# Row factors turned in 32x32 blocks, low parts stacked in the last key block, score tiles halved across two banks

## What is computed

```python
scores = scale * np.matmul(q, k.transpose(0, 1, 3, 2))      # 4 batches x 8 heads, 576 x 576, D = 64
a = np.exp(causal(scores) - rowmax); a /= a.sum(-1) + 1e-09
local = np.matmul(a, v)
mem_ret  = np.einsum('bhsd,bhde->bhse', phi(q), M_prev)      # phi(x) = where(x > 0, x, exp(x) - 1) + 1
mem_norm = np.einsum('bhsd,bhd->bhs', phi(q), z_prev) + 1e-6
x = g * mem_ret / mem_norm + (1 - g) * local                # g = sigmoid(beta), one number per head
x = act1(x @ w_in1) @ w_out1                                # 2304 tokens, 512 -> 2048 -> 512
x = act2(x @ w_in2) @ w_out2                                # the same shape again
```

## Time and profile before

| | us |
|---|---|
| runs | 1031.84, 1031.50, 1033.06 |
| median | 1031.84 |
| profiled execution | 1034.39 |
| its span | 1032.6 |
| slots 0 to 5 (no dense layer) | 0 to 53.7 |
| slots 6 to 32, attention and first layer | 53.7 to about 528 |
| dense layers alone | about 528 to the end |
| granted TensorE clock, mean | 0.996 |

### The profile page before, as it was taken

How to read it: one execution, slowest core, us unless ns; L and a number is a source line. 1 busy time by engine, 2 the same in 40 slices (tenths; PEclk the granted TensorE clock), 3 DMA queues, 4 the chain that set the end, 5 groups by cost and what they waited for, 6 DMA issues and landing times.

```text
span 1032.6 us, 16556 instructions
## 1 busy us (share of the span) xinstructions
PE 1011.8 (98%) x6158; PEld 873.2 (85%) x6158; DVE 432.8 (42%) x1091; ACT 526.6 (51%) x1144; POOL 425.4 (41%) x380
## 2 busy tenths in 40 slices
PE   7889999999999999999999999999999999999997
PEld 4668888989898898988999998888888888888896
DVE  6677756656555655556531337212121211211111
ACT  6668777777676766767643456222222222322221
POOL 3367746455546455464532258322222222222211
PEclk9999999999999999999999999999999999999999
DMA  5655333323322322322201066000200200100010
GB/s 142 166 167 175 56 85 63 79 63 71 87 58 61 85 69 67 78 61 74 62 15 42 22 220 188 1 21 1 62 21 0 62 21 1 37 25 1 1 41 21
DMA packets 96272, 66.34 MB, mean 64 GB/s; under 512 B 72064, under 2 KB 85824, under 8 KB 96192
## 3 DMA queue, kind: packets, MB, share of 16 engines
q1 hardware_dynamic: 95328, 62.14, 23.4%
q10 hardware_dynamic: 864, 3.15, 1.0%
HBM read 54.53 MB, written 10.66 MB: 63 GB/s over the span
## 4 chain that ended last, share of the span: by engine, by line
PE 87%; POOL 1%; issue 0%; DVE 0%; POOLq 0%; ACT 0%
PE Hp L630 13%; PE Hp L631 12%; PE Hp L632 12%; PE Yp L653 7%; PE Yp L655 6%; PE Yp L654 6%; PE At L654 6%; PE At L655 6%; PE At L653 6%; PE At L570 5%; PE At L545 4%; PE At L494 4%; PE At L530 1%; PE At L582 0%; POOL WAl L1219 0%
## 5 line engine op out<-in xcount | busy, mean ns | idle before, releaser
L1224 POOL TENSOR_TENSOR Gl<-Gl_raw,Gh 128x512 fp32r<-128x512 f32 x144 | 191.7, 1331 | 425.7 <-ACT Gh L869 425.7
L630 PE MATMUL Hp<-Xh,WAh 128*128 128x256 f32 (+1 forms) x704 | 217.5, 309 | 1.3 <-POOL WAl L1219 1.3
L631 PE MATMUL Hp<-Xl,WAh 128*128 128x256 f32 (+1 forms) x704 | 212.5, 302 | 0.0
L632 PE MATMUL Hp<-Xh,WAl 128*128 128x256 f32 (+1 forms) x704 | 212.5, 302 | 0.0
L1085 DVE TENSOR_TENSOR Gl_raw<-Hp,Gl_raw 128x512 f32<-128x512 f32 x72 | 49.8, 692 | 296.4 <-ACT Gl_raw L861 296.3
L861 ACT ACTIVATE Gl_raw<-Hp 128x512 f32<-128x512 f32 x72 | 43.1, 598 | 230.5 <-PE Hp L632 230.5
L630 PEld LDWEIGHTS Hp<-Xh,WAh 128*128 128x128 f32 x704 | 133.2, 189 | 12.8 <-issue 2.0
L869 ACT ACTIVATE Gh<-Gl_raw 128x512 fp32r<-128x512 f32 x144 | 91.0, 632 | 99.1 <-DVE Gl_raw L1085 52.3
L631 PEld LDWEIGHTS Hp<-Xl,WAh 128*128 128x128 f32 x704 | 133.3, 189 | 6.8
L632 PEld LDWEIGHTS Hp<-Xh,WAl 128*128 128x128 f32 x704 | 133.4, 189 | 5.0
L653 PE MATMUL Yp<-WBh,Gh 128*128 128x512 f32 x320 | 133.3, 417 | 2.8 <-POOL Gl L1224 2.8
(11 more groups left out here) (144 smaller groups left out, 1933.5 us busy)
## 6 DMA issues: line engine op xcount, KB each, us to landing
raw<-long SPq DMA_DIRECT2D x16, 480.0 KB, 4.5
WAl_raw<-w_in SPq DMA_DIRECT2D x13, 512.0 KB, 5.3
WBl_raw<-w_out SPq DMA_DIRECT2D x13, 512.0 KB, 4.2
Vs_raw<-vv SPq DMA_DIRECT2D x16, 320.0 KB, 3.4
yT_scratch<-xraw SPq DMA_DIRECT2D x36, 128.0 KB, 2.5
prob<-yT_scratch SPq DMA_DIRECT2D x9, 512.0 KB, 4.2
out<-prob SPq DMA_DIRECT2D x36, 128.0 KB, 2.2
raw<-short SPq DMA_DIRECT2D x11, 384.0 KB, 4.4
```

The source lines that it names most:

```text
L630: pe.matmul(h, WAh[:, f, j, :], xh, start=(j == 0), stop=False)
L631: pe.matmul(h, WAh[:, f, j, :], xl, start=False, stop=False)
L632: last = pe.matmul(h, WAl[:, f, j, :], xh, start=False, stop=(j == DT - 1))
L1224: gp.tensor_tensor(Gl[:, U % 2, :], act[:, U % 2, :], Gh[:, U % 2, :].bitcast(F32), ALU.subtract).then_inc(g_lo, 1)
```

## The change

Three edits, independent of each other.

First, `turn_sums` and `sums_out` go, with the wait of TensorE's head-1 transposes on `rt_out`. `rnr` becomes 32 columns wide (the upper 16 are zero), and `factors` itself, right after the gating, turns it in four blocks of 32x32 on DVE into `rt`, now 32 partitions by 128. `send_sums` moves on SP from tick 3 of the next slot (in the opening: the head of the next slot) to behind `send_norms`, at tick 7 of the work's own slot. Second, in the last key block of each head (64 keys) the low part of the turned exponentials is written to partitions 64 to 127 of `PTh`, the values carry those 64 keys twice, and one matmul with 128 rows does for two. DVE's group with that block becomes two instructions. The values come in two arrays with the duplicated block in place. Third, part 1's two tiles are each cut in two equal halves, one in each bank: 288 + 288 and 224 + 224 columns, in place of 512 + 64 and 448; `row_max` reads a tile through a pattern over both banks.

```diff
-    [(448, 576, 0, 0, (2, 5)), (320, 448, 576, 640, (1, 4))],
+    [(448, 576, 0, 0, (2, 5)), (320, 448, 288, 640, (1, 4))],
@@ def both_heads, scores (TensorE)
-                for q0, width, col, _, _ in TILES[part(n)]:
-                    first = min(width, 512 - col % 512)
-                    last = both_heads(n, q0, 0, first, col)
-                    if first < width:
-                        last = both_heads(n, q0, first, width - first, col + first)
+                for q0, width, col, _, _ in TILES[part(n)]:
+                    if part(n) == 0:
+                        last = both_heads(n, q0, 0, width, col // BANK, col % BANK)
+                    else:
+                        for bank in range(2):
+                            last = both_heads(n, q0, bank * width // 2, width // 2, bank, col)
@@ def transposes (TensorE)
-                    pe.wait_ge(rt_out, n)
@@ def values (TensorE)
-                    pe.wait_ge(pt_lo, weights_before(b) + 2 * h + 2)
+                    pe.wait_ge(pt_lo, low_before(b) + 3 * h + 3)
-                        for pt in (PTh, PTl):
+                        for pt in (PTh, PTl) if cols != HALF_BLOCK else (PTh,):
@@ TensorE, ScalarE
-            def turn_sums(b):
-                pe.wait_ge(rn_gated, b + 1)
-                pe.transpose(At[0:6, 0, 512 - P:512], rnr[:, 0:6], ident[:, :]).then_inc(rt_done, 1)
-            def sums_out(n):
-                sc.wait_ge(rt_done, n + 1)
-                after(sc, sums_sent, 16 * n)
-                sc.activation(rt[:, :], At[0:6, 0, 512 - P:512], ACT.Copy).then_inc(rt_out, 1)
@@ def weights_low (VectorE)
+                    whole = cols - i * HALF_BLOCK
-                    ve.tensor_tensor(PTl[:, h, dst:dst + cols], At[:, bank, src:src + cols], ...
+                    ve.tensor_tensor(PTl[:, h, dst:dst + whole], At[:, bank, src:src + whole], ...
+                    if i == 1:
+                        c, d = slice(src + whole, src + cols), slice(dst + whole, dst + cols)
+                        ve.tensor_tensor(PTh[HALF_BLOCK:P, h, d], At[0:HALF_BLOCK, bank, c], PTh[0:HALF_BLOCK, h, d].bitcast(F32),
+                                         ALU.subtract).then_inc(pt_lo, 1)
@@ def factors (VectorE), k = 7
+                ve.wait_ge(rn_gated, n + 1)
+                for i in range(P // BLOCK):
+                    p = slice(BLOCK * i, BLOCK * i + BLOCK)
+                    ve.transpose(rt[:, p], rnr[p, :]).then_inc(rt_out, 1)
@@ def slot (SyncE)
-                if k == 3 and back is not None:
-                    send_sums(back)
                 if k == 7 and front is not None:
                     send_norms(front)
+                    send_sums(front)
```

More of the change, by code:

```diff
@@ L151, in stores, with build @@
     return 128 * min(i - CHUNKS + 1, TWOS) + (64 if i == LAST else 0)
-def build(nc, short, long, vv, beta, wa1, wb1, wa2, wb2, out):
+def build(nc, short, long, v_short, v_long, beta, wa1, wb1, wa2, wb2, out):
     left_dram = nc.dram_tensor("left_scratch", [PAIRS, P, TAIL], F32).ap()
@@ L198, in build @@
         gates = sb("gates", [P, 2, H])
[L199 removed]
+        rn, rnr, rt = sb("rn", [P, RN]), sb("rnr", [P, BLOCK]), sb("rt", [BLOCK, P])
         rn_tiny, rn_gate = sb("rn_tiny", [P, RN]), sb("rn_gate", [P, H // 2, RN])
@@ L241, in score_bank, with score_tile, as_score @@
             bank = At[:, 2 * h:2 * h + 2, :] if n >= OTHER_BANKS else (Hp, Yp)[h][:, :, :]
-            return bank.rearrange("p a c -> p (a c)")
+            return bank
+        def score_tile(n, h, i):
+            _, width, col, _, _ = TILES[part(n)][i]
+            if part(n) == 1:
+                return score_bank(n, h)[:, :, col:col + width // 2]
+            return score_bank(n, h)[:, col // BANK, col % BANK:col % BANK + width]
+        def as_score(n, ap):
+            return ap.rearrange("p (a c) -> p a c", a=2) if part(n) == 1 else ap
         def odd(n):
@@ L336, in load_v @@
                 after(sp, pv_done, n - 1 if n < PLAIN else values_before(n))
-                sp.dma_start(v_place(n)[:, 0:j, :, 1, :], vv[pair(n), :, 0:j]).then_inc(v_in[odd(n)], 16)
+                sp.dma_start(v_place(n)[:, 0:j, :, 1, :], (v_short, v_long)[part(n)][pair(n)]).then_inc(v_in[odd(n)], 16)
             def cut_norms(n):
@@ L493, in both_heads @@
                         r = slice(D * h, D * h + D)
-                        last = pe.matmul(score_bank(n, h)[:, col:col + width], qt[r, q0:q0 + P], kt[r, k0:k0 + width],
+                        last = pe.matmul(score_bank(n, h)[:, bank, col:col + width], qt[r, q0:q0 + P], kt[r, k0:k0 + width],
                                          start=(step == 0), stop=(step == len(steps) - 1))
@@ L568, in values @@
                         vs = Vs[:, j, h, :, :].rearrange("p a d -> p (a d)")
-                        for pt in (PTh, PTl):
+                        for pt in (PTh, PTl) if cols != HALF_BLOCK else (PTh,):
                             last = pe.matmul(At[:, 2 + h, col:col + cols], vs, pt[:, h, src:src + cols],
-                                             start=(j == 0 and pt is PTh), stop=(j == len(blocks) - 1 and pt is PTl))
+                                             start=(j == 0 and pt is PTh), stop=(j == len(blocks) - 1))
                     last.then_inc(pv_done, 1)
@@ L591, in slot @@
                     if front is not None:
-                        after(pe, pt_lo, weights_before(front - 1))
+                        after(pe, pt_lo, low_before(front - 1))
                         if front >= OTHER_BANKS:
                             pe.wait_ge(max_done, tiles_before(front) + NT[part(front)])
-                    if back is not None:
-                        turn_sums(back)
                     if front is not None:
@@ L1105, in _ @@
             ve.memset(rn[:, :], 1.0).then_inc(zeroed, 1)
+            ve.memset(rnr[:, RN:BLOCK], 0.0).then_inc(gates_laid, 1)
             ve.memset(rn_tiny[:, 0:6], 1e-9).then_inc(gates_laid, 1)
@@ L1266, in second, with values @@
         return np.ascontiguousarray(w.reshape(UNITS, 2, P, DM).transpose(0, 2, 1, 3).reshape(UNITS, P, 2 * DM))
-    v = np.concatenate([v.reshape(HEADS, S, D), np.zeros((HEADS, 5 * P - S, D), v.dtype)], axis=1)
+    def values(keys):
+        w = v.reshape(HEADS, S, D)
+        w = np.concatenate([w[:, 0:keys], w[:, keys - HALF_BLOCK:keys]], axis=1)
+        return np.ascontiguousarray(w.reshape(PAIRS, 2, -1, P, D).transpose(0, 3, 2, 1, 4))
     M = M_prev.reshape(PAIRS, 2, D, D)
@@ L1274 @@
         "long": rows(1),
-        "vv": np.ascontiguousarray(v.reshape(PAIRS, 2, 5, P, D).transpose(0, 3, 2, 1, 4)),
+        "v_short": values(KEYS_IN[0]), "v_long": values(KEYS_IN[1]),
         "beta": np.ascontiguousarray(beta),
```

37 lines of the change are left out of this document (19 added, 18 removed).

## The result

The changed kernel took 1026.45 us (median of 5 runs, 1026.04 to 1027.86); beside it the kernel before took 1031.84 (5 runs, 1031.50 to 1035.05). The ratio is 0.9942, 95% interval 0.9926 to 0.9959: faster, by 5.4 us where 12.1 were forecast. The profiled execution took 1026.56 us, its span 1024.8.

A forecast was written before the change was run, and what follows sets the result against it. TensorE, busy 98% of the span, was taken to bound the kernel. Terms 5.3 + 2.8 + 2.5 + 1.5 = 12.1 us gave 1022.3 against the profiled execution, 1019.7 against the median; range 1016.2 to 1023.8.

The forecast's parts named there:

- the three steady terms: TensorE's stream: stacked low parts save 5.3 us, halved score tiles 2.8, the turn taken off TensorE 2.5.
- Rival B: Streamed columns, not weight loads, pace TensorE's short matmuls: 5.6 us gained, 1026.2; chance 0.05.
- the covers late: From slot 10 on, DVE's idle time of about 2.2 us a slot hides the transposes; output matmuls hide the extra low part.
- F: Rival: TensorE waits 0.2 us in each `values` for the extra low part; 7.3 us gained, 1024.5; chance 0.03.
- the transposes: Four 32x32 transposes a slot on DVE, running end to end, take 0.75 us, within 0.4 to 1.0.
- Rival E: Slower: the transposes wait for POOL's access to SBUF, 0.92 us each; 1060 if nothing else hid it; chance 0.04.
- The opening and slots 6 to 9: Early slots: 1.5 us gained together, with ends of 2.5 lost and 5 gained.
- Slot 1: Opening: slot 1 pays 0.75 us, as the next phi stands behind the factors on DVE.
- Slots 7 to 9: DVE goes into the row maxima without idle time in slots 7 and 8; the transposes' 0.75 comes out there, -0.8.
- The 2.0 for an earlier factor DMA and a warmer clock: Slots 5 and 6: SP's factor DMA comes over 1.0 us earlier, cutting TensorE's wait and cold clock; 2.0 of 3.8 us.
- The 0.3 for the opening: Slots 1 to 5: TensorE's 6.1 us of waits for `rnr` go, but what follows is late; 0.3 us gained.
- Rival C: Parts 1 to 3 as priced, but the early slots lose 2.5 us: 8.1 gained, 1023.7; chance 0.13.

The follow-up runs named there:

- e2: The kernel before with the stacked low parts and halved tiles only, the turn staying on TensorE; 1023.92 us, ratio 0.9921.
- e8: The changed kernel with the four transposes made twice for every work from 10 on, the second time into an unread tile; 1026.61 us.
- e3: The changed kernel with only work 0's four transposes moved behind phi_sum(1) on VectorE; 1023.55 us, ratio 0.9914.
- e6: Against e5: in slot 0 phi_sum(1) goes ahead of all of factors(0); 1021.11 us, ratio 0.9892.
- e11: Trace execution of the changed kernel with the transposes of works 6, 7 and 8 made twice; that kernel's median is 1028.79 us.
- e5: The changed kernel with work 0's transposes behind phi_sum(1) and those of works 5 and up in the next slot; 1020.97 us, ratio 0.9893.
- e4: The changed kernel with every work's transposes moved to the next slot, the sums sent at tick 3 again; 1022.49 us, ratio 0.9906.
- e7: The changed kernel with GpSimd's first split of WA held until phi_sum(1) is done; 1025.37 us, ratio 0.9936.
- e12: Against e6: VectorE's first split of WB put behind plain_weights(0) in slot 1; 1020.53 us, ratio 0.9881.

## Why the prediction was wrong

**Right: the three steady terms.** 5.3 + 2.8 + 2.5 = 10.6 were forecast, 10.8 came. The low parts gave 0.25 a slot where two loads of 0.11 were taken; the tiles 0.15 where 0.18; the turn 0.10 to 0.12 where 0.11. Rival B (columns pace the short matmuls) is out; that its 1026.2 lies nearest to the 1026.45 measured is luck. It has 1.6 us from the low parts and the tiles, where e2 measured 8.1, and a gain of 1.5 in the early slots, where 5.4 were lost. The Trainium skill (TensorE: Matmul & The Clock Gate, "Back-to-back issue gap") with its 81 ns would have made 3.9 us of the 5.3, as an estimate; e2's 0.25 us for two heads is 0.12 for each load and its matmul, so the trace disagrees with it for these operands, and the row of loads was the better price.

**Right: the covers late.** The extra low part (0.22 us each) made TensorE wait nowhere from slot 10 on, so F is out. The transposes hide, even doubled (e8).

**Right in kind, small in size: the transposes.** I took 0.75 us within 0.4 to 1.0. The group's row in the changed kernel:

```profile
L970 DVE STREAM_TRANSPOSE rt<-rnr 32x32 f32<-32x32 f32 x128 | 25.6, 200 | 4.1
```

200 ns each, end to end, and 0.93 us for four to the next start. Rival E (they wait for GpSimd) is out: beside its split they took 0.89 in e3.

**Wrong: "The opening and slots 6 to 9".** The step that failed is the sum 0.3 + 2.0 - 0.8 = 1.5 us gained. The traces show 3.0 lost. By the medians it is more: the profiled execution of before lay 2.55 above its median, and since the time from slot 10 on is the same to 0.1 us in all the kernels that share it, I take this excess to lie ahead of slot 10 too. That is worked out and not seen, for there is one trace of before. So slot 10 starts at about 122.7 us in a median execution of before (123.0 to 123.6 by its later medians) and at 128.1 in one of after: 5.4 lost (4.5 to 5.1 by the later ones). With the gain of 1.5 that I had forecast this is 6.9, and less the 0.2 by which the late part came out better it is the miss, 1026.45 - 1019.7 = 6.8. By its terms:

- Slot 1 was priced at 0.75. It cost 2.9 (e3): 0.93 of transposes, `phi_sum` at 1.87 in place of 0.48, and a longer stretch at 1.2 GHz. I had put "phi stands behind the factors" in the sum and not asked what else starts on the same signal: `rn_gated` also releases GpSimd's split. Part of it is the clock. From the memory product's start to the scores of work 2 pass 21.94 - 15.56 = 6.38 us in the changed kernel, at 1.2 GHz for most of it, and 18.47 - 11.49 - 0.43 - 1.83 = 4.72 in e6 (less its two waits), at full clock: 1.7 us, an estimate from two executions. In e8 and e11, whose code is that of the changed kernel up to here, the 6.38 is 6.04 and 7.06.
- Slots 7 to 9 were priced at the 0.75 once, -0.8. They cost 2.6 (e5 against e3): the row maxima of works 7, 8 and 9 each stood right behind the transposes, and the full length counts every time.
- The 2.0 for an earlier factor DMA and a warmer clock did not come. I said that this DMA would be issued over 1.0 us earlier than 48.60; it is at 48.15. The wait for `Gl` in slot 6 did go, and so did the cold stretch of the earlier trace rows, but a stretch at 1.2 GHz from 50.6 to 54.0 stood in its place, and work 10 starts where VectorE's chain lets it. In e2 the wait for `Gl` was 0.3 us with nothing done to it. In e4, with the transposes out of the way, it was 1.94. So I take it for a matter of the single execution, where I had taken it for a property of the kernel; one trace of each does not show it.
- The 0.3 for the opening: with the transposes out of the way (e5) slot 10 starts at 122.6 by the median, in e2 at 122.9. The 6.1 us of waits for `rnr` were worth nothing, since what follows was late by as much. In slot 1 the turn's wait and the memory product's wait end on neighbouring instructions of VectorE.

Rival C had the right mechanism, the early slots lose, but with 2.5 as its price where 5.4 came; it had 0.13 of the chances and should have been the forecast. The range ended at C's 1023.8 because I bounded slot 1 by the transposes' length. What the opening's waits hand on to one another from slot 3 to 5 I did not separate.

## What to carry over

Work that goes from a full engine to one with 42% busy time is free only where that engine idles behind it: read the stretches one by one, above all those where its instructions stand without gaps, and put the new work behind whatever the next engine waits for. A wait that is removed is worth the distance to the next late result, not its length. And before a gain is read off a wait in one execution, compare that execution's time with the median: here it lay 2.55 us above, more than the 2.0 that I wanted to gain from its wait and its clock.

## What the runs showed of the hardware

**Some instructions of VectorE wait for GpSimd's to end, those with two SBUF inputs above all.** `phi_sum(1)` started at 13.63 and ended at 15.50, 0.34 behind the split's end (12.82 + 2.34 = 15.16). In e7 VectorE's weight split (1.22 alone) ran from 15.24 to 17.19, and GpSimd's ended at 16.10. The gating L965 (0.18 us alone) ended at 93.96, with GpSimd's split ending at 93.93. Each ended as if it had started 0.13 to 0.15 us ahead of GpSimd's recorded end and then taken its usual time. If VectorE's started first, it kept its time (12.21 against 12.44 in e3: 0.49), and GpSimd's took 2.48 in place of 2.34. The reciprocal (0.25) and the transposes (0.89 for four), with one input, took the same time beside GpSimd as alone. But one input does not free an instruction as such. The TENSOR_SCALAR of phi takes 0.32 us alone (at 17.24 in e12), and in slot 2 of e6, beside GpSimd's, 0.83, ending 0.19 behind it:

```profile
23.36 0.83 DVE L985 TENSOR_SCALAR phi<-Rh_raw 128x320 f32<-128x320 f32 x1
...
23.14 0.86 POOL L1191 TENSOR_TENSOR xt<-xt,bc 128x320 f32<-128x320 f32 x1
```

The Trainium skill says so (SBUF — State Buffer, "SBUF: two separate sides"): VectorE and GpSimd share a pair of ports, held for a whole instruction by the one that starts first, and VectorE wants it for operations with two SBUF inputs, against a GpSimd operation that reads SBUF, and for those in a two-port mode. The traces agree in each case with two inputs; whether the TENSOR_SCALAR runs in such a mode no run here shows. The rule would have pointed at slot 1 beforehand.

**In the traces kept here, what differs between executions lies early.** From slot 10 to the end the kernels with all three edits took 896.5 or 896.6 us in nine traces, though these executions lay from 1.1 us below (e6) to 1.8 above (e12) their kernels' medians. The changed kernel, e8 and e11 have the same code up to slot 6, and work 2 started at 21.94, 21.43 and 22.54 in them, with 6.8, 3.4 and 6.8 us at 1.2 GHz between 12 and 22 us. The start of slot 10 moved by 2 us between kernels that differ by one instruction's place (121.60 in e6, 123.91 in e12), where the stretch at 1.2 GHz around 47 to 54 us lasted 3.4 us in the one and 6.8 in the other.
